# A fused attention and two mixture-of-experts layers on one core: decay table, first loads and routing reordered

## The reference

```python
# attention: B=4, H=8, S=768, D=48; per head a decaying state
for t in range(S):
    cur = einsum('bhd,bhe->bhde', u * k[t], v[t])
    y[t] = einsum('bhd,bhde->bhe', r[t], state + cur)
    state = w[:, :, None] * state + einsum('bhd,bhe->bhde', k[t], v[t])
# x: 3072 rows of 384.  first layer of 8 experts, rows with x @ w_skip <= 0 pass unchanged
e = argmax(x @ w_gate); g = softmax(x @ w_gate)[e]
x = x + g * (relu(x @ w1[e]) @ w2[e])
# second layer of 8 experts, all rows, no residual, weights of its own
out = g2 * (relu(x @ w1b[e2]) @ w2b[e2])
```

## Time and profile before

| what | us |
|---|---|
| median of the runs | 594.86 |
| lowest and highest | 594.35, 595.63 |
| the profiled execution | 589.84 |
| its span, first to last instruction | 588.1 |
| TensorE busy | 539.8 (92%) |
| DVE busy | 387.9 (66%) |
| ACT, POOL busy | 251.9, 249.9 |

### The profile page before, as it was taken

How to read it: one execution, slowest core, us unless ns; L and a number is a source line. 1 busy time by engine, 2 the same in 40 slices (tenths; PEclk the granted TensorE clock), 3 DMA queues, 4 the chain that set the end, 5 groups by cost and what they waited for, 6 DMA issues and landing times. The chain is left out here.

```text
span 588.1 us, 16050 instructions
## 1 busy us (share of the span) xinstructions
PE 539.8 (92%) x5550; PEld 512.8 (87%) x5551; DVE 387.9 (66%) x839; ACT 251.9 (43%) x704; POOL 249.9 (42%) x348
## 2 busy tenths in 40 slices
PE   3999999988799999999857879999999999999992
PEld 3899998978699999999855769999999999999992
DVE  5888888867688878888613927463747464647330
ACT  0233333334077667776413017362736352626220
POOL 5887778742244444454410043232534323324331
PEclk9999999997899999999969989999999999999997
DMA  9798888876187777776378014544444534111100
GB/s 140 121 188 165 161 161 162 169 254 224 43 312 223 209 230 250 244 236 212 60 245 304 0 54 115 185 157 147 139 165 153 162 140 147 50 46 43 39 15 26
DMA packets 114127, 89.58 MB, mean 152 GB/s; under 512 B 80672, under 2 KB 104931, under 8 KB 114080
## 3 DMA queue, kind: packets, MB, share of 16 engines
q1 hardware_dynamic: 106304, 74.16, 45.1%
q0 software_dynamic: 7776, 14.82, 9.1%
HBM read 80.44 MB, written 13.27 MB: 159 GB/s over the span
## 5 line engine op out<-in xcount | busy, mean ns | idle before, releaser
L822 DVE TENSOR_TENSOR w_lo<-w_raw,w_hi 128x384 fp32r<-128x384 f32 (+1 forms) x224 | 130.2, 608 | 4.7 <-ACT w_hi L817 3.1
L1092 PE MATMUL e_ps_h<-e_x_hi,w_hi 128*128 128x192 f32 (+3 forms) x384 | 119.6, 311 | 3.2 <-DVE e_x_lo L1210 2.9
L817 ACT CAST w_hi<-w_raw 128x384 fp32r<-128x384 f32 (+1 forms) x224 | 119.9, 566 | 3.8 <-issue 3.5
L1094 PE MATMUL e_ps_h<-e_x_hi,w_lo 128*128 128x192 f32 (+3 forms) x384 | 119.6, 311 | 0.0
L1093 PE MATMUL e_ps_h<-e_x_lo,w_hi 128*128 128x192 f32 (+3 forms) x384 | 119.5, 311 | 0.0
L1250 DVE SCALAR_TENSOR_TENSOR e_h_lo<-e_ps_h,e_h_hi 128x128 fp32r<-128x128 f32 (+1 forms) x192 | 70.5, 396 | 44.5 <-ACT e_h_hi L1179 40.1
L1092 PE MATMUL e_ps_y<-w_hi,e_h_hi 128*128 128x384 f32 x272 | 95.5, 351 | 0.0
L1094 PE MATMUL e_ps_y<-w_hi,e_h_lo 128*128 128x384 f32 x272 | 91.5, 336 | 0.0
L1093 PE MATMUL e_ps_y<-w_lo,e_h_hi 128*128 128x384 f32 x272 | 91.1, 335 | 0.0
L1092 PEld LDWEIGHTS e_ps_h<-e_x_hi,w_hi 128*128 128x128 f32 x384 | 72.9, 190 | 5.4 <-DVE e_x_lo L1210 3.4
L1094 PEld LDWEIGHTS e_ps_h<-e_x_hi,w_lo 128*128 128x128 f32 x384 | 72.9, 190 | 1.2
(11 more groups left out here) (168 smaller groups left out, 922.4 us busy)
## 6 DMA issues: line engine op xcount, KB each, us to landing
w_raw<-in_moe_w_dram SPq DMA_DIRECT2D x32, 1536.0 KB, 7.3
r_in<-in_r_dram SPq DMA_DIRECT2D x24, 192.0 KB, 3.2
k_in<-in_k_dram SPq DMA_DIRECT2D x24, 192.0 KB, 3.9
v_in<-in_v_dram SPq DMA_DIRECT2D x24, 192.0 KB, 4.0
x_rows<-rows SPq DMA_DIRECT2D x24, 192.0 KB, 3.5
w_lo<-x_rows SPq DMA_DIRECT2D x6, 768.0 KB, 6.6
x_in<-x_rows,e_ent_in POOLq DMA_INDIRECT x33, 3.1
out_dram<-y_rows,e_ent_out POOLq DMA_INDIRECT x19
```

The lines of the kernel that those rows point to most:

```text
L817: act.copy(self._of(self.hi1[par], self.hi2[par], n), self._of(self.raw1[par], self.raw2[par], n)).then_inc(self.hi_done[par], 1)
L822: eng.tensor_tensor(self._of(self.lo1[par], self.lo2[par], n), self._of(self.raw1[par], self.raw2[par], n), self._of(self.hi1[par], self.h ...
L1092: pe.matmul(o, s_hi, m_hi, start=(k == 0), stop=False)
L1094: return pe.matmul(o, s_lo, m_hi, start=False, stop=(k == last))
```

## The change

It has seven parts.

1. **Loads at the start.** w goes straight to `w_pow` and is loaded, with u, from ACT's queue; SP starts with r, k and v. POOL clears only the padding of `r_in` and `k_in`. r and k have a semaphore of their own (`rk_loaded`), v another (`v_loaded`).
2. **The decay table.** `shrink` is made on POOL by doubling from 1 (six products and one more), beside DVE's `grow`; the copy of w, the reciprocal and the product on DVE go; `shrink_up` comes after the first `rk`.
3. **The first step.** TensorE does the scores of step 0, then the table's transposes, and only then r and k of step 1; DVE masks step 0 ahead of `rk` of step 1.
4. **Loads of x for the second routing.** The first load of four tiles becomes two of two tiles; three groups of four tiles, not four, are issued at the end of the experts' stage, and the fourth in the routing.
5. **TensorE between the stages.** 16 identity transposes at the start of the second routing go, and 72 stand at the end of the first layer of experts.
6. **Routing.** ACT writes the row numbers' part of `col_hot` (24 products) in place of DVE's two instructions; in the first routing it stands between ACT's sixth and seventh piece of weights. `e_iota` is made first and has a semaphore of its own. In the second routing, ACT's and DVE's code is put in a loop of one turn whose first instruction is placed at the start of a block of 256 instruction slots (`head_slot`).
7. **The end.** SP, not POOL, waits for the last scatters.

The core of the diff:

```diff
-            sp.wait_ge(dve_zeroed, 2)
-            for j in range(2):
-                sp.dma_start(w_col[PAD * j:PAD * j + D, :], w.rearrange("(n j) d -> j d n", j=2)[j], allow_slow_non_contiguous=True).then_inc(small, 16)
-            sp.dma_start(u_row[:], u.rearrange("h d -> (h d)").partition_broadcast(P)).then_inc(small, 16)
...
                 for dst, src in ((r_in, r), (k_in, k)):
-                    sp.dma_start(dst[b][:, :, 0:D], src[b, :, bass.ds(t0, P), :].rearrange("h t d -> t h d")).then_inc(loaded[b], 16)
-                sp.dma_start(v_in[b][:], v[b, :, bass.ds(t0, P), :].rearrange("h t d -> t h d")).then_inc(loaded[b], 16)
+                    sp.dma_start(dst[b][:, :, 0:D], src[b, :, bass.ds(t0, P), :].rearrange("h t d -> t h d")).then_inc(rk_loaded[b], 16)
+                sp.dma_start(v_in[b][:], v[b, :, bass.ds(t0, P), :].rearrange("h t d -> t h d")).then_inc(v_loaded[b], 16)
...
-                pool.memset(r_in[n][:], 0.0).then_inc(zeroed, 1)
-                pool.memset(k_in[n][:], 0.0).then_inc(zeroed, 1)
+                pool.memset(r_in[n][:, :, D:PAD], 0.0).then_inc(zeroed, 1)
+                pool.memset(k_in[n][:, :, D:PAD], 0.0).then_inc(zeroed, 1)
...
+            pool.memset(shrink[:, :, HALF - 1:HALF], 1.0).then_inc(shrunk, 1)
+            for n in range(6):
+                m = 2 ** n
+                pool.wait_ge(shrunk, n + 1)
+                pool.wait_ge(tables, POWERS[n])
+                pool.tensor_tensor(shrink[:, :, HALF - 2 * m:HALF - m], shrink[:, :, HALF - m:HALF], w_pow[:, n, :].unsqueeze(2).to_broadcast([P, NP, m]), ALU.mult).then_inc(shrunk, 1)
+            pool.wait_ge(shrunk, 7)
+            pool.wait_ge(tables, LOW)
+            pool.tensor_tensor(shrink[:, :, HALF:P], shrink[:, :, 0:HALF], grow[:, :, 0:1].to_broadcast([P, NP, HALF]), ALU.mult).then_inc(shrunk, 1)
...
+            pool.wait_ge(tables, TABLE_STEPS)
...
+            act.wait_ge(dve_zeroed, 1)
+            for j in range(2):
+                act.dma_start(w_pow[PAD * j:PAD * j + D, 0, :], w.rearrange("(n j) d -> j d n", j=2)[j], allow_slow_non_contiguous=True).then_inc(w_loaded, 16)
+            act.dma_start(u_row[:], u.rearrange("h d -> (h d)").partition_broadcast(P)).then_inc(u_loaded, 16)
...
-            link(dve.reciprocal(shrink[:, :, 0:P // 2], grow[:, :, 1:P // 2 + 1]))
-            link(dve.tensor_tensor(shrink[:, :, P // 2:P], shrink[:, :, 0:P // 2], grow[:, :, 0:1].to_broadcast([P, NP, P // 2]), ALU.mult))
-            link(dve.tensor_tensor(shrink_up[:], shrink[:], w_pow[:, 7, :].unsqueeze(2).to_broadcast([P, NP, P]), ALU.mult))
...
+            dve.wait_ge(shrunk, 8)
             rk(0, 0)
+            dve.tensor_tensor(shrink_up[:], shrink[:], w_pow[:, 7, :].unsqueeze(2).to_broadcast([P, NP, P]), ALU.mult).then_inc(tables, 1)
...
-                if not last:
+                begins = isinstance(i, int) and i == 0
...
+                if not last and not begins:
...
+                if begins:
 
...
-            pe.wait_ge(tables, TABLE_STEPS)
-            for p in range(NP):
-                ins = pe.transpose(ps_x[:, P * p:P * p + P], shrink_up[:, p, :], ident[:])
-            ins.then_inc(tab_ps, 1)
...
+                    pe.wait_ge(tables, TABLE_STEPS + 1)
+                    for p in range(NP):
+                        ins = pe.transpose(ps_x[:, P * p:P * p + P], shrink_up[:, p, :], ident[:])
+                    ins.then_inc(tab_ps, 1)
+                    turn_rk(0, 1)
...
+    src = x_rows.rearrange("(b c p) d -> c p b d", b=dst.shape[1], p=P)[g]
+    if g == 0:
+
+        for n in range(2):
+            eng.dma_start(dst[:, 2 * n:2 * n + 2, :], src[:, 2 * n:2 * n + 2, :]).then_inc(x_loaded[n], 16)
+    else:
+        eng.dma_start(dst, src).then_inc(x_loaded[g + 1], 16)
...
+        def from_line_start(eng):
+
+            return nc.Fori(0, 1, engines=[eng.engine], head_slot={eng.engine: 0}) if TURN else nullcontext()
...
-                for g in range(len(x_in), TILES // GRP):
-
-                    sp.wait_ge(x_turned, GRP * (g - len(x_in) + 1))
+                for g in range(len(x_in) - 1, TILES // GRP):
+
+                    if g >= len(x_in):
...
+            pool.iota(e_iota[:], [[1, E]], base=0, channel_multiplier=0, allow_small_or_imprecise_dtypes=True).then_inc(e_made, 1)
...
-                stay_warm(pe, ident, ps_xT[0][:, 0:P], 2)
...
-                    pe.wait_ge(ids_placed, 2 * n // PLACES + 1)
                     pe.wait_ge(gates_placed, 2 * n // PLACES + 1)
+                pe.wait_ge(ids_placed, n + 1)
...
+            with from_line_start(act):
...
+                if not TURN:
+                    for n in range(W.N1):
+                        W.hi(act, 0, 0, n)
+                act.wait_ge(id_made, 1)
+                for place in range(PLACES):
+                    if place % (PLACES // 2) == 0:
+                        act.wait_ge(col_equal, 2 * place // PLACES + 1)
+                    for i in range(GP * place, GP * place + GP):
+                        ins = act.mul(col_hot[:, i, 0, :], col_is[:, i, :], entry[:, i, 0:1])
+                    ins.then_inc(ids_placed, 1)
+                if not TURN:
+                    for n in range(W.N1, W.N):
...
-                if n:
-                    dve.wait_ge(ids_placed, n)
-                    dve.wait_ge(gates_placed, n)
-                dve.tensor_tensor(col_is[:], row_iota[:, 0:NCOL].unsqueeze(1).to_broadcast(wide),
-                                  col_i[:, i].unsqueeze(2).to_broadcast(wide), ALU.is_equal).then_inc(col_equal, 1)
...
-                dve.wait_ge(id_made, 1)
-                dve.tensor_tensor(col_hot[:, i, 0, :], col_is[:], entry[:, i, 0].unsqueeze(2).to_broadcast(wide), ALU.mult).then_inc(ids_placed, 1)
...
+            end = sp.value_load(starts[0:1, E:E + 1], min_val=1, max_val=top)
+
+            sp.wait_ge(scattered, 16 * (end + 1))
+            if m == 0:
                 load_next(sp)
+            else:
+
+                sp.sem_inc(all_stored, 1)
...
-            end = pool.value_load(starts[0:1, E:E + 1], min_val=1, max_val=top)
...
-            if m == 1:
-                pool.wait_ge(scattered, 16 * (end + 1))
...
+                stay_warm(pe, ident, ps_h[0][:, 0:P], 9)
...
-            for g in range(len(bulk)):
+            for g in range(len(bulk) - 1):
...
```

216 lines of the change are left out of this document (113 added, 103 removed).

## The result

The changed kernel takes 586.29 us (median of 4 runs, 585.44 to 588.29) against 594.61 for the kernel before (4 runs, 594.03 to 595.63): a ratio of 0.9863, 95% interval 0.9835 to 0.9892, so 8.3 us faster. The prediction was 586.8. The profiled execution of the changed kernel took 586.31 us, on the median, with a span of 584.3. (A span goes from the first to the last instruction, and is 1.6 to 2.1 us shorter than the time.)

The account below looks back on a forecast made before the run. TensorE, busy nine tenths of the span, bounds the expert layers; gains lie around them. Terms 2.0 + 0.3 + 0.4 + 3.1 + 1.3 + 1.0 = 8.1 us off the 594.86 median give 586.8, range 582.5 to 591.0.

Parts of the forecast that it names:

- Start: Attention's start: earlier r and k and a quicker decay table bring `k_end` from 16.61 to 14.5; 2.0 us, range -0.4 to +2.8.
- right behind the identity transposes: Attention's first step: scores run at 12.0 to 13.1 (1.10 us), directly after the identity transposes and before the table's.
- First routing: First routing: DVE's 0.33 wait for POOL's constants goes, ACT ends last at 152.6; gain 0.3 us, between 2.4 lost and 1.2 gained.
- Hand-over: Between first experts and second routing: TensorE turns x near 301.5 instead of 304.1; 0.4 us taken, between -1.0 and +1.3.
- stall: Second routing: ACT's 4.78 us gap before 319.28, read as code arriving late, goes; 3.1 us, at most 3.8.
- the packet that it pointed at: Second routing: one 16 KB instruction packet among full DMA queues between 315 and 320, cited for ACT's code arriving late.
- the second rival: Second routing: ACT's branch at 300.3 must fetch its block, hand-over -0.3 instead of +0.4, stall still goes; 587.5 us, chance 0.10.
- 72 transposes: End of first experts: they fill TensorE and hold its clock, taking 8.3 to 9.5 us; just fit or cost up to 1.0.
- Places in the second routing: Second routing: DVE loses two products, second-half `row_hot` comes earlier, TensorE's 1.00 wait goes; 1.3 us, range -0.7 to +1.4.
- Second experts: Second expert layer: only TensorE's own work counts and the change leaves that alone; no term in the sum.
- End: After the last scatter: POOL's read and wait move to SP, cutting the 7.8 us tail; 1.0 us taken, near the low end.

Follow-up runs that it names:

- second profile of before: The kernel before, unedited, run again and profiled in an execution nearer its median: 594.38 us, span 592.7.
- experiment 6: The changed kernel with the first step's old order (table transposes and step 1's r and k ahead of the scores): 585.55 us, ratio 0.9828 to before.
- experiment 5: The kernel before with only empty one-trip loops on ACT and DVE at the end of the first experts: 588.92 us, ratio 0.9922.
- experiment 2: The changed kernel without the one-trip loops around ACT's and DVE's second-routing code: 584.94 us, ratio 0.9864 to before.
- experiment 3: The changed kernel with empty one-trip loops at the end of the first experts instead of those around the routing code: 584.57 us, ratio 0.9855 to before.
- experiment 10: The changed kernel without the 72 transposes at the end of TensorE's first experts: 586.81 us, ratio 0.9876 to before.
- experiment 9: The changed kernel with the row-number products back on DVE instead of ACT's 24, in both routings: 587.15 us, ratio 0.9890 to before.
- experiment 8: The changed kernel with the wait for the last scatters back on POOL instead of SP: 588.63 us, ratio 0.9911 to before.

## Why the prediction was right, and where it was not

The time was right (586.8 against 586.29), and the sum too (8.1 against 8.3 in the medians and 8.4 between the second profile of before and after). The terms were not all right: the start (3.13 at the first routing) and the end gave 2.5 us more than forecast and the first experts 0.55 more, hand-over and stall gave 1.7 less and the second experts 0.9 less. That these nearly cancel is luck.

- **Start, 2.0 predicted.** The mechanism held, with two errors inside it that cancel. TensorE's first turn came at 7.30, not at 6.6: k was issued at 1.74 as forecast, but landed later. And the 16 identity transposes took 2.90 us at the upper clock level, not 3.62 at the lower. So they ended at 11.94 (11.9 predicted); scores at 11.86, `k_end` at 14.26 (14.5 predicted), the sum at 18.13 (18.5). POOL's table ended at 7.76 (7.5). w came at 4.71, not at 3.5, but DVE's chain of powers and `grow` took 4.1 us and not 6.5, so this was covered. Against the first profile of before it is 2.37 at the second rows. Against the second it is 3.82, since 1.45 of a low clock stretch goes too, a term which the prediction did not have. At the first routing 3.13 are left. What failed is one step: the sum puts the scores (1.10) "right behind the identity transposes" and ahead of the table without asking whether that order gains. It loses 0.8 (experiment 6), though the prediction had named `k_end` as the link on which the pace hangs.
- **First routing, 0.3.** ACT was last, as predicted, and ended at 151.26 with products of 0.23 us each (0.25). From `m_top` to the gathers 0.65 was gained (19.65 to 19.00); by the first product 0.05 on the first profile of before and 0.21 on the second, since the identity transposes behind the gathers ran at a low clock.
- **Hand-over and stall, 0.4 and 3.1.** Together 1.78. The stall was what the prediction took it for (experiment 5: 26.31 to 22.42, 3.9 us with the place of the code alone), but the packet that it pointed at, 16 KB on q8, is not the sign of it; the 8 KB on q14, which the same view has, is (experiment 2). In the changed kernel the loops were not needed for it: without them there is no gap either (experiment 2). The step that failed is the argument against the second rival, that ACT "has nothing to do for over 10 us ahead of the branch, time for a block to come". It did not come: ACT and DVE started at 303.76 and 304.18. The entry pays, and 1.7 us of it count, more than the 0.7 of that rival. DVE was late as well, and TensorE's clock fell in the wait (0.57 from 304 to 308), so the third group was turned 12.5 us after the issue of the loads, where the prediction had 10.1 and experiment 2 has 10.9; what each of the two adds no run parts. Without the loops the stage gives 26.31 - 22.87 = 3.44, near the 3.5 predicted. By the Trainium skill ("Runtime: NRT & Kernel Launch", section "Instruction fetch mechanics") a taken branch to a block outside the window waits for the fetch of it; experiments 2 and 3 agree (3.8 and 3.9 us with the branch beside full queues, none without it). Its other rule, that crossing into the next block is mostly hidden, does not always hold here beside full queues, if the gap of 4.78 and 4.89 us was such a crossing, as its going with the place of the code suggests. The two later packets of the kernel after (experiment 2), which delay nothing, agree with it.
- **72 transposes.** Predicted 8.3 to 9.5 us; they took 8.02, at the full clock, and fitted. (The 8.47 it scaled from is the time of 62 transposes, not 64, as the row says; this changed nothing.) What they gain is not shown (experiment 10).
- **Places in the second routing, 1.3.** 1.27, and experiment 9 gives the same part alone as 1.26. This term was right; ACT's products kept up (2.79 us for 12).
- **Second experts, 0.** A loss of 0.70 up to the last scatter, all of it in the clock: the kernel after has 6 us at 0.50 in the first products. It is no loss of the change: before has 228.03 and 230.07 us in its two profiles, after 230.77, and experiment 8, with the same code there, 228.04.

```profile
346.00:352.00 6.00, 4.97 (x16) 4.98 (x17) 1.36 (x3) 1.26 (x4) 2.68 (x5) 0.50 0.12 34
```

- **End, 1.0.** 2.3, by the profiles and by experiment 8. The size was off: it was taken near the low end of its bounds, and lay in the middle.

Sum of what was found: 3.13 + 0.21 + 0.55 (first experts, up to the loads of x) + 1.78 + 1.27 - 0.88 (to the last scatter: -0.18 and -0.70) + 2.34 = 8.40.

## What to carry to other kernels

When a profiled execution lies off the median of the timed runs, profile the kernel again before reading differences of a few microseconds from it: here more than half of the gain was not in the first pair of profiles.

A gap with no cause in the profile, on an engine that runs while the transfer queues are full, can be code arriving. A packet on an instruction queue inside the gap is a hint; that the gap goes when only the code's place changes is the proof. Move the jump to the code, with an empty loop, to a time when the engine is idle and the queues are not full; the same jump made inside the full stretch gives back nearly half.

A change that is a gain as a whole can carry parts that lose. Three of them, undone together, gave some 4 us more. The place to look is the link which the whole chain hangs on, and what now stands ahead of it in its engine's queue.

## What the runs showed of the hardware

- Entering a one-trip loop at a block start held ACT and DVE for 3.8 and 3.9 us while the queues moved 364 GB/s (their first copies came 7.77 and 8.19 us after the issue of the loads with it, 3.98 and 4.31 without); the same loop run at low traffic (37 GB/s from 286 to 297) held nobody.
- The granted clock falls to 0.50 at different places in executions of one kernel; twelve runs of the kernel before have mean clocks between 0.959 and 0.975 and spans between 588.2 and 593.4. A low stretch around the second table is in 13 of 14 profiles, and costs the second experts' products 1.5 to 2.8 us where it reaches into them.
- Two transfers of 384 KB instead of one of 768 KB let TensorE start on the first tiles 1.2 us sooner, and on the next 768 KB 0.3 to 1.6 us later.
- The wait for the last scatters ended the program 2.3 us sooner on SP than on POOL, which had issued them (6.48 to 6.56 against 8.76 to 8.86 us from the last issue).
